# Attention, a routed expert layer and a feed-forward layer in one kernel: an expert weight load moved into the head loop, VectorE's routing moved inside its steps, ScalarE's squares and casts behind its last copy, and a reordered setup

## What is computed

```python
scores = scale * q @ k.T                       # 4 batches, 8 heads, 576 tokens, 64 wide
decay = cum[:, :, :, None] - cum[:, :, None, :]    # cum: running sum of log(clip(f))
scores = where(causal, -1e9, scores + decay)
attn = softmax(scores);  x = attn @ v          # x: 2304 tokens x 512
logits = normalized(x) @ normalized(expert_emb).T / tau
expert = argmax(logits); gate = softmax(logits)[expert]
h = relu(x[mask] @ w1[e]);  y[mask] = gate * (h @ w2[e])     # 8 experts, 512 -> 1024 -> 512
out = softplus(y @ w_in) @ w_out               # 512 -> 2048 -> 512
```

## Time and profile before

| | us |
|---|---|
| runs | 955.76, 950.84, 950.36 |
| median | 950.84 |
| profiled execution | 955.27 |
| its span, first to last instruction | 953.50 |
| TensorE busy | 928.8 (97%) |
| VectorE, ScalarE, GpSimd busy | 541.9, 404.2, 334.3 |
| attention (to the first matmul of an expert, L1518) | 274.55 |

### The profile page before, as it was taken

How to read it: one execution, slowest core, us unless ns; L and a number is a source line. 1 busy time by engine, 2 the same in 40 slices (tenths; PEclk the granted TensorE clock), 3 DMA queues, 4 the chain that set the end, 5 groups by cost and what they waited for, 6 DMA issues and landing times.

```text
span 953.5 us, 17188 instructions
## 1 busy us (share of the span) xinstructions
PE 928.8 (97%) x5380; PEld 829.2 (87%) x5381; DVE 541.9 (57%) x1403; ACT 404.2 (42%) x694; POOL 334.3 (35%) x275
## 2 busy tenths in 40 slices
PE   8899999979999999999999999999999999999997
PEld 5899999979887788888888889899898999899896
DVE  8577779959765645555565554444343443444433
ACT  7576778737444313013331533333333333333331
POOL 6365564343306867446877520100100100100101
PEclk9999999979999999999999999999999999999999
DMA  5865655565246665525676110000000100000000
GB/s 153 200 165 132 191 133 115 120 220 118 66 176 210 235 203 195 191 87 177 220 251 211 40 39 12 34 23 12 34 23 12 44 11 11 33 0 0 34 1 34
DMA packets 55917, 99.25 MB, mean 104 GB/s; under 512 B 23416, under 2 KB 23416, under 8 KB 55360
## 3 DMA queue, kind: packets, MB, share of 16 engines
q1 hardware_dynamic: 38368, 49.62, 19.1%
q10 hardware_dynamic: 14592, 39.59, 12.6%
q0 software_dynamic: 2912, 9.46, 2.7%
HBM read 80.88 MB, written 17.75 MB: 103 GB/s over the span
## 4 chain that ended last, share of the span: by engine, by line
PE 88%; DVE 4%; issue 2%; DMA 2%; ACT 1%; another core or an unknown queue 1%; SPq 1%; POOL 1%; POOLq 0%; DVEq 0%
PE ps L1648 21%; PE ps L1661 21%; PE ps L1589 11%; PE ps L1569 10%; PE ps L1410 10%; PE ps L1394 5%; PE ps L1371 4%; PE ps L1578 2%; PE ps L1427 1%; PE ps L1347 1%; PE ps L1518 1%; PE ps L1635 1%; PE ps L1551 1%; DMA vT_ring<-vT 1%
## 5 line engine op out<-in xcount | busy, mean ns | idle before, releaser
L1661 PE MATMUL ps<-W,ghl 128*128 128x512 f32 x864 | 215.3, 393 | 0.0
L556 POOL TENSOR_TENSOR W<-raw,W 128x512 fp32r<-128x512 f32 x144 | 181.5, 1301 | 84.3 <-ACT W L778 84.3
L1648 PE MATMUL ps<-yTh,W 128*128 128x384 f32 x768 | 197.6, 338 | 0.0
L1661 PEld LDWEIGHTS ps<-W,ghl 128*128 128x128 f32 x864 | 160.4, 188 | 30.4 <-issue 0.8
L1290 DVE SCALAR_TENSOR_TENSOR sp_a<-ps,sp_a 128x384 f32<-128x384 f32 x96 | 53.5, 557 | 207.7 <-ACT sp_a L812 207.7
L808 ACT ACTIVATE sp_a<-ps 128x384 f32<-128x384 f32 x96 | 47.3, 493 | 250.8 <-PE ps L1648 250.8
L594 POOL DMA_INDIRECT out<-out_sb,out_row x18 | 17.3, 964 | 377.6 <-DVE out_sb L1309 375.4
L1648 PEld LDWEIGHTS ps<-yTh,W 128*128 128x128 f32 x768 | 139.9, 188 | 6.9
L778 ACT CAST W<-raw 128x2048 fp32r<-128x2048 f32 x36 | 67.4, 1909 | 174.3 <-issue 57.2
L1410 PE MATMUL ps<-v_ring,pT_sb 128*128 128x100 f32 x960 | 130.0, 279 | 4.8 <-DVE lgh L925 3.2
L1648 PE MATMUL ps<-yTl,W 128*128 128x384 f32 x384 | 129.4, 337 | 0.0
(11 more groups left out here) (274 smaller groups left out, 1249.8 us busy)
## 6 DMA issues: line engine op xcount, KB each, us to landing
raw<-w ACTq DMA_DIRECT2D x25, 1024.0 KB, 5.4
qk_raw<-qkT SPq DMA_DIRECT2D x64, 288.0 KB
ys_dram<-y_sb SPq DMA_DIRECT2D x21, 256.5 KB, 5.3
x_raw<-xs_dram SPq DMA_DIRECT2D x19, 257.0 KB, 3.0
vT_ring<-vT SPq DMA_DIRECT2D x16, 288.0 KB, 4.5
v_ring<-v SPq DMA_DIRECT2D x32, 128.0 KB, 4.0
first_raw<-w ACTq DMA_DIRECT2D x4, 1024.0 KB, 5.8
raw<-w_in ACTq DMA_DIRECT2D x4, 1024.0 KB, 5.2
```

Of the source, the lines that this page charges most:

```text
L556: pool.tensor_tensor(wcols(par, 1, c)[:, p], RAW[c][:, p], wcols(par, 0, c)[:, p].bitcast(F32), ALU.subtract).then_inc(wl_done, 1)
L1648: ins = pe.matmul(bank(f_ % 2, GN), W[:, a:a + P], y[par][:, c, :], start=(m == 0), stop=(m == 3 * DC - 1))
L1661: ins = pe.matmul(bank(2 + k), ghl[:, (f_ + 2) % 4, part, k * P:k * P + P], W[:, a:a + DM], start=(f_ == 0 and m == 0), stop=(f_ == FC2 - ...
```

## The change

- **The load.** ScalarE's 1 MB load in step 24 is gone. In its place `second_half_load` sits in the head loop behind the last copy of step `s == 8`, so that heads 8 and 16 each load one half (512 KB) into the same buffer.
- **VectorE's routing.** `early_routing` moves from ahead of `normalize` to between `evac(h-1, 0)` and the last `maxima`. `place` is split: `offsets(1)` is done in step 27, `positions(1)` stays near the end of step 28, `next_base(1)` goes to step 29; `square_sums(1)` moves up within step 27. The sum over eight heads becomes a sum over seven ahead of `normalize` (`seven_heads`) and an addition behind it. TensorE's `ranks` moves up to match.
- **ScalarE.** `evac(h-1, 3)` goes ahead of the squares, of the weight load and of the cast; one square per step is done behind the first `probs`. `norms` and `exps` come one step earlier.
- **Setup.** The second `vT` load is issued right behind the first; head 0's row of `k2` is loaded from ScalarE's queue; the first casts of head 2 move up on VectorE and ScalarE in step 1; GpSimd sets 36 instead of 100 columns of `v_ring` and writes `zeros` between heads 2 and 3; the wait for `v_ones` leaves the sync engine.

Both `vT` loads stand together ahead of head 3's q and k. The diff, cut to its core:

```diff
 @block.sync
-                if s % 2 == 0:
+                if s % 2 == 0 and (late or h > 2):
...
-                sp.dma_start(k2[2:4, h, :].bitcast(F32), row).then_inc(first_loaded[h], 16)
+                if h == 1:
+                    sp.dma_start(k2[2:4, h, :].bitcast(F32), row).then_inc(first_loaded[h], 16)
...
                     load_vT(0, 0)
+                    load_vT(1, 1)
...
-            sp.wait_ge(v_ones, 1)
 @block.gpsimd
-                pool.memset(v_ring[:, :, :, :], 1.0).then_inc(v_ones, 1)
-                pool.memset(zeros[:, :], 0.0).then_inc(zeros_set, 1)
+                pool.memset(v_ring[:, :, :, D:VN], 1.0).then_inc(v_ones, 1)
+                pool.wait_ge(v_ones, 1)
+                pool.memset(v_ring[64:P, :, NB - 1, 0:D], 0.0).then_inc(v_ones, 1)
...
-            for h in range(2, 4):
-                low_qk(h, h % 2, 1)
+            low_qk(2, 0, 1)
+            pool.memset(zeros[:, :], 0.0).then_inc(zeros_set, 1)
+            pool.wait_ge(zeros_set, 1)
+            low_qk(3, 1, 1)
 @block.scalar
-            SQUARES = {TAIL: range(0, 4), TAIL + 1: range(4, 7), TAIL + 2: range(7, 10), TAIL + H: range(10, 13), TAIL + H + 1: range(13, 15)}
+            SQUARES = {TAIL: range(1, 4), TAIL + 1: range(5, 8), TAIL + 2: range(9, 10), TAIL + H: range(11, 14)}
+            SQUARE = {TAIL: 0, TAIL + 1: 4, TAIL + 2: 8, TAIL + H: 10, TAIL + H + 1: 14}
...
+            def second_half_load(i):
+
+                act.dma_start(RAW[0][:, bass.ds(i * F1, F1)].rearrange("p (o f) -> p o f", o=1),
+                              w1[1:2, bass.ds(i * P, P), :].rearrange("o p f -> p o f")).then_inc(raw_loaded[0], 16)
+
             def act_step(h, s):
+                if isinstance(h, int) and h == 1:
+                    scale_k(0, 1)
                 if has(h, 0, NH):
                     probs(h, s, [0])
...
+                if in_tail(h) and h in SQUARE:
...
+                    square_block(SQUARE[h])
+                if has(h, 1, NH + 1):
+                    evac(h - 1, s - 1, 1)
...
-                if isinstance(h, int) and h in (22, 28):
+                if isinstance(h, int) and h in (21, 27):
                     norms((h - TAIL) // H)
...
                     high_k(h + 2, s, (h + 2) // 2 if isinstance(h, int) else batch[0] * 4 + (s + 2) // 2)
+                if has(h, 1, NH + 1):
+                    evac(h - 1, s - 1, 3)
+                if in_tail(h):
                     for j in SQUARES.get(h, []):
                         square_block(j)
-                    if h == 24:
-                        src, dst = expert_chunk(1, 0)
-                        act.dma_start(dst, src).then_inc(raw_loaded[0], 16)
                 if not isinstance(h, int):
                     first_weights(batch[0], s - 2)
-                if has(h, 1, NH + 1):
-                    evac(h - 1, s - 1, 3)
+                if not isinstance(h, int) and s == 8:
+                    second_half_load(batch[0])
...
-            high_k(0, 0, 0)
+            scale_k(0, 0)
+            act.wait_ge(rows_set, 1)
+            act.wait_ge(cum_ready, 3)
+            act.dma_start(k2[2:4, 0, :].bitcast(F32), cum_hl[0:1, :, :].bitcast(F32)).then_inc(first_loaded[0], 16)
+            round_k(0, 0)
...
-                    act.wait_ge(raw_loaded[c], turn * 16)
+                    act.wait_ge(raw_loaded[c], turn * 16 + (16 if c == 0 else 0))
 @block.vector
+            def seven_heads(h):
+
+                first = (h - (H - 1)) * NB // H if isinstance(h, int) else loop_block(h)
+                dve.wait_ge(x_ready, h)
+                nv.tensor_reduce(batch_logits(h, first), lgh[:, 0:H - 1, :, :].rearrange("p h b e -> p b e h"),
+                                 AX.X, ALU.add).then_inc(lg_part, 1)
...
-                    nv.tensor_reduce(lg.rearrange("p e b -> p b e"), lgh[:, :, :, :].rearrange("p h b e -> p b e h"),
-                                     AX.X, ALU.add).then_inc(lg_sum, 1)
+                    dve.wait_ge(lg_part, turn_of(h) + 1)
+                    nv.tensor_tensor(lg, lg, lgh[:, H - 1, :, :], ALU.add).then_inc(lg_sum, 1)
...
                 if h == 27:
                     count_before(1)
+                    square_sums(1)
+                    offsets(1)
                 if h == 28:
-                    place(1)
                     shift(1)
                 if h == 29:
                     gate(1)
+                    next_base(1)
...
             def dve_step(h, s):
                 if has(h, 0, NH):
                     maxima(h, s, [0, 1])
+                if isinstance(h, int) and h == 1:
+                    dve.wait_ge(qk_loaded[0], 64)
+                    dve.wait_ge(scores_ready, NU)
+                    round_q(0)
                 if has(h, 1, NH + 1):
                     evac(h - 1, s - 1, 0)
+                if in_tail(h):
+                    early_routing(h)
                 if isinstance(h, int) and h == 1:
                     turned_embeddings()
-                    high_q(2, 0, 1)
+                    copy_q(0)
...
-                if in_tail(h):
-                    early_routing(h)
+                if isinstance(h, int) and h == 28:
+                    positions(1)
+                if (s - 2) % H == H - 1 and not (isinstance(h, int) and not 2 <= h < NH):
+                    seven_heads(h - 2)
                 if has(h, 2, NH + 2):
                     normalize(h - 2, s - 2)
...
-                if isinstance(h, int) and h == 27:
-                    square_sums(1)
 @block.tensor
+                if st and h in RANKS:
+                    ranks(RANKS[h])
                 if turn:
                     transposes(h - 1, s - 1, 1)
...
-                if st and h in RANKS:
-                    ranks(RANKS[h])
```

More of the change, by code:

```diff
@@ L904, in evac, with turn_of, batch_logits @@
                 nv.tensor_copy(pT_sb[:, s % 2, a:b], bank(4, b - a)).then_inc(ptD, 1)
+            def turn_of(h):
+                return h // H if isinstance(h, int) else batch[0]
+            def batch_logits(h, first):
+                second = isinstance(h, int) and h >= 2 * H
+                lg = ROUTE[1]["lg"][:, :, :] if second else ROUTE[0]["lg"][:, :, bass.ds(first, NB)]
+                return lg.rearrange("p e b -> p b e")
+            def seven_heads(h):
[3 more added lines that the diff above has]
+                                 AX.X, ALU.add).then_inc(lg_part, 1)
             def normalize(h, s):
@@ L1020, in place, with offsets @@
             def place(g):
+                offsets(g)
+                positions(g)
+                next_base(g)
+            def offsets(g):
                 t, q = parts(g)
-                lo, hi = GROUP_BLOCKS[g]
                 first = t["before"][:, :, 0]
@@ L1030, in place, with next_base @@
                 then(nv.tensor_copy(pos[:, lo:hi], q["posf"]))
-                then(nv.tensor_tensor(q["count"], t["run"][:, :, hi - lo - 1], first, ALU.subtract))
+            def next_base(g):
+                t, q = parts(g)
+                lo, hi = GROUP_BLOCKS[g]
+                then(nv.tensor_tensor(q["count"], t["run"][:, :, hi - lo - 1], t["before"][:, :, 0], ALU.subtract))
                 then(nv.tensor_tensor(q["base"], q["count"], region[:, :] if g == 0 else ROUTE[g - 1]["base"][:, :], ALU.add))
@@ L1403, in times_v @@
                         pe.wait_ge(ve_ready, (h // 2 if isinstance(h, int) else pair_of(h, s)) + 1)
-                    if not (isinstance(h, int) and h < 1):
+                    if isinstance(h, int) and h < 1:
+                        pe.wait_ge(v_ones, 2)
+                    else:
                         pe.wait_ge(x_ready, h)
```

46 lines of the change are left out of this document (27 added, 19 removed).

## The result

| | before | changed |
|---|---|---|
| runs | 11 | 11 |
| median, us | 952.0 (949.96 to 964.96) | 945.41 (944.81 to 959.25) |
| ratio | | 0.9927, interval 0.9912 to 0.9942 |
| profiled execution, us | 955.27 | 944.81 |
| attention, to the first matmul of an expert | 274.55 | 265.29 |

The change makes the kernel 0.7% faster, 6.6 to 7 us: clear of its interval, but less than the 1% that the forecast had set as its bound, and less than half of the 15 us that it forecast (936.0, range 929 to 946). One run of each kernel, 964.96 and 959.25 us, fell into a slower state and is left out of the ratio. The mechanism that happened is the first rival: the load is innocent, and the stall D is still there. The median lies within the range only because the range took in the upper end of that rival.

A forecast was written before the change was run, and what follows sets the result against it. TensorE is fully busy from 320 us, so only attention can change; 4.7 + 1.5 + 1.4 + 8.9 + 2.5 = 19.0 us off 955.27 gives 936.3 profiled. Off the median, 14.6 gives 936.2; forecast 936, range 929 to 946.

The forecast's parts named there:

- the first rival: Step 25: the load is innocent, scatters make the stall; the rest gains 10.1 us, to 945.2 or 940.7; chance 0.2.
- D: Step 25, 10.9 us too long beside load and scatters: removing the load gains 8.9 us (0 to 10.9).
- step from trace to median: Profiled execution 4.4 us over the median: difference put into step 25, so a normal run gains 14.6, to 936.2 us.
- A: Setup, step 2: earlier second `vT` load removes TensorE's 2.72 us wait and the low clock; gains 4.7 us (2.7 to 5.8).
- B: Head loop, steps 5 to 17: copy ahead of cast and the shortened sum gain 1.5 us (0.5 to 1.7).
- rival 4: Half loads stall steps 8 and 16, 2 to 4 us each, giving 942 us; chance 0.04.
- C: Steps 18 to 21: ScalarE's copy ahead of squares and routing moved gain 1.4 us (-1 to 1.9).
- E: Steps 26 to 29: less of `place` and `shift` ahead of `normalize` gains 2.5 us (0 to 4).
- Nothing should give it back: Expert stage: starts sooner by the whole 19.0 us, its chains all starting from attention's end, so the gain stays.
- Rival 3: Steps 18 to 23 and 26 to 29: routing inside the step costs 2.5 us each; 965 or 960.7 us; chance 0.06.
- Rival 2: Only A and D gain, VectorE and ScalarE still late in C and E: 15.1 us, to 940.2; chance 0.12.

The follow-up runs named there:

- experiment with ScalarE's order: Changed kernel with ScalarE's last copy put back behind the squares and the cast of weights; 949.16 us in its one execution.
- kernel with landed bursts: Changed kernel with scatters in bursts of 3, 3, 2, 2, then 3 and 2, each landed before the next; 935.99 us (ratio 0.9949) and 935.23 us (0.9815).

## Why the prediction was wrong, step by step

**D failed, and with it the forecast.** The step was: "I take it that load and scatters together make the 10.9 us and that the scatters alone leave about 2, near the 2.41 us of the bare scatter." The load made nothing of it (17.40 us without it), and the scatters alone make all (6.71 us without them). Two readings led there. "The large wait starts with the load" took nearness in time for cause; that the first scatters cause nothing was right, but it is a mark of scatters: in these traces two or three in a row cost nothing and longer rows do. And the 2.41 us was one wait of ScalarE with five scatters, in one trace, taken as the price of ten. It measured neither what TensorE loses nor what more scatters do. Even with five the three other traces of the kernel before have 3.66 to 3.80 us there, and TensorE idle for 0.80 to 0.95 us; in the changed kernel it is idle for 1.42 to 1.60. The rival had the right mechanism. That its time off the trace, 945.2, is what the profiled execution took (944.81) is partly luck, by what follows. Its chance was also stated in two ways: "most of it above 941.3", but the 0.81 for faster needs 0.11 of its 0.2 below.

**The step from trace to median failed too.** "I put that difference into D, the one place that looks irregular." The 4.4 us lay in step 2, where the clock falls in some executions after the wait for `vT`, in step 29 and in the wait for `x_raw`. D's step 25 is 17.44 to 17.64 us in all four traces of the kernel before. This matters for A: of the 3.8 us that it gains against the profiled execution, only 0.4 is left against one that took 949.91 (head 4's scores at 37.03 there, 36.68 now). Up to head 30's scores the changed kernel gains 10.8 us on the one execution and 5.7 on the other. It is why 10.5 us between the traces are 6.6 to 7 between the medians, and why the rival's 940.7 off the median was too low. The changed kernel's runs lie closer together: ten of the eleven within 3.3 us.

**A, 3.8 of 4.7.** The wait for `vT` and the low clock went, and the scores of head 3 stand at 29.18 as forecast. `copy_q` beside GpSimd took 1.20 us, as its twin's 1.27 had said. What I had missed are the loads that come next. Head 4's decay rows are issued at 29.59, 0.7 us later than before, and take 6.97 us to land, while TensorE arrives 4 us sooner; it waits 0.56 us, and step 3 takes 7.50 us instead of 6.72. In the second trace of the changed kernel step 3 is undisturbed, but now the third `vT` is late, and step 4 takes 8.70 us instead of 7.85. From the chain of the first trace and TensorE's timeline of the second:

```profile
29.59 6.97 DMA k<-cum_dram
```

```profile
41.10 1.36 PE L1495 MATMUL ps<-enb,vT_ring 128*128 128x100 f32 x10 [0.60 <-DMA vT_ring<-vT]
```

I had looked at q and k of head 3 alone. Step 3 varies from 6.72 to 7.95 us in the traces of the changed kernel and its variants, step 4 from 7.83 to 8.78. Whether the earlier second `vT` makes these loads slow was not tested.

**B, 1.2 of 1.5, and as reasoned.** 0.53 and 0.54 in steps 8 and 16 are the copy ahead of the cast, as the experiment with ScalarE's order shows; 0.16 is step 10, which kept its 8.35 us in that experiment; I put it down to the sum over seven heads, which no run has alone. I had taken nearly all of the 0.67 there; 0.5 stays. The half loads cost nothing: steps 8 and 16 take 7.84 us, which ends rival 4.

**C and E, 1.9 of 1.4 and 3.6 of 2.5.** I had kept back 0.5 and 1.7 us for squares, routing and conversions that come late; of step 19's excess nothing is left but the rank matmuls. In E 1.5 of the gain is step 29's low clock, which the other traces of before don't have in that length, so the lasting gain is 2.1. Rival 3, the broken rhythm, did not come true in the changed kernel, but something like it exists: with ScalarE's copy late and the routing in its new place, steps 19 and 20 take 0.8 us more each than before. Rival 2 is refuted by the gains in C and E, and by D.

**The expert stage.** "Nothing should give it back" came out within 0.3 us, but by two errors that cancel: 10.8 us earlier at head 30, 9.3 at the first expert matmul, 10.5 at the end. The 1.5 us were lost beside the five scatters, where the changed kernel waits 1.42 us and this trace of the kernel before does not wait; 1.1 of the 1.2 us that came back are the wait for `x_raw` at 314.07, which the changed kernel's trace doesn't have.

## What to carry to other kernels

When several transfers surround a stall, move each alone before pricing the removal of one: the load that starts beside a wait may be a bystander. Before a change is taken off a median, find in two traces where the runs differ, because a gain in the part that varies is worth only its share. In this kernel indirect scatters were better issued in short bursts that land before the next than ten in a row; the price is what GpSimd owes to TensorE and what queues behind the wait.

## What was not expected of the hardware

- Long runs of indirect scatters from GpSimd (one every 1.27 us) hold up TensorE. VectorE and ScalarE wait 6 to 12 us, in part for matmuls that the trace shows as finished, and in most of the traces TensorE itself stands still for nothing that the profile shows (4.0 us in six gaps, 7.41 us in one). Ten in a row cost TensorE 10.6 us with the low clock that follows, six cost 6, five up to 1.6 us of idleness, and three or two that land in between nothing measurable. No other transfer is needed for it. What in them does it was not settled.
- The stall seems to be a matter of the chip or its state; as each session had a chip of its own, the two can't be told apart. In two of five sessions the kernel before took 941 to 942 us instead of 951 to 953, and fifteen scatters in a row left no such wait, where the same fifteen had made one of 12.4 us. The difference is about what the stall costs, but neither kernel of the pair was traced there, so that it is D that is missing is only argued. The kernel with landed bursts took 935 to 936 us in both kinds of session.
- The low clock behind a wait in step 2 comes or not with 1.8 us more or less of that wait: 2.72 us idle in one trace (then eight matmuls in 1.92 us), 0.90 us in another (1.06 us).
